# Attention on one Trainium2 core: in even chunks the sum of turns, its rounding and its phases move forward, and GpSimd's tally is cut in two

## What is computed

```python
mag = np.sqrt(a_re * a_re + a_im * a_im)
scale = np.minimum(mag, 0.999) / (mag + 1e-06)
a_re_n, a_im_n = (a_re * scale, a_im * scale)
for t in range(S):                                   # B, H, S, D = 4, 8, 768, 48
    new_re = ar * S_re - ai * S_im                   # ar, ai: a_re_n, a_im_n at t
    new_im = ar * S_im + ai * S_re
    kv = np.einsum('bhd,bhe->bhde', k[:, :, t], v[:, :, t])
    S_re, S_im = (new_re + kv, new_im)
    y[:, :, t] = np.einsum('bhd,bhde->bhe', q[:, :, t], S_re)
...
e_idx = np.argmax(x @ w_gate, axis=1)                # x: y by token, for the experts
eom = 1.0 / (1.0 + np.exp(-(x @ w_output_gate)))     # scales the chosen expert's output
```

## Time and profile before

| | |
|---|---|
| median of 3 runs | 978.09 us (977.53 to 978.83) |
| the profiled execution: its own time | 978.09 us |
| its span in the trace | 976.3 us |
| attention, in the trace | to about 290 us |
| experts and feed-forward | from there to the end |
| PE busy | 940.3 us, 96% of the span |
| DVE, ACT, POOL busy | 438.7, 441.9, 510.1 us |
| granted TensorE clock | 0.996 of full |

### The profile page before, as it was taken

The page is one execution under the profiler, slowest core; times in us unless marked ns, Lnnn a source line. Parts: engine busy times, 40 slices in busy tenths (PEclk is TensorE's granted clock), DMA queues, the critical chain, the costliest instruction groups (busy, mean ns, idle before and its releaser), DMA issues.

```text
span 976.3 us, 18188 instructions
## 1 busy us (share of the span) xinstructions
PE 940.3 (96%) x5904; PEld 836.7 (86%) x5905; DVE 438.7 (45%) x794; ACT 441.9 (45%) x742; POOL 510.1 (52%) x429
## 2 busy tenths in 40 slices
PE   5999999999879999999999999999999999999997
PEld 4777878887877989989999898999998999999997
DVE  5898898898846333433433432222222122222111
ACT  7999888997711222222222333333333333333322
POOL 4134656656464986767759923343243433423433
PEclk9999999999989999999999999999999999999999
DMA  3642363340153645335355520010010000000000
GB/s 121 205 139 83 113 238 99 101 137 2 64 183 94 205 133 167 113 105 169 113 169 169 130 57 17 9 41 17 9 49 17 29 21 17 33 1 1 33 1 32
DMA packets 74123, 83.89 MB, mean 86 GB/s; under 512 B 57653, under 2 KB 63305, under 8 KB 71497
## 3 DMA queue, kind: packets, MB, share of 16 engines
q1 hardware_dynamic: 67048, 47.20, 17.5%
q0 software_dynamic: 6144, 34.65, 10.2%
q10 hardware_dynamic: 864, 1.19, 0.3%
HBM read 65.59 MB, written 17.38 MB: 85 GB/s over the span
## 4 chain that ended last, share of the span: by engine, by line
PE 77%; ACT 10%; DVE 5%; issue 5%; DMA 1%; POOL 1%; ACTq 1%; SPq 0%; POOLq 0%; DVEq 0%
PE bank L2168 21%; PE bank L2181 20%; PE bank L2156 12%; PE bank L2131 12%; PE bank L2141 3%; PE bank L1098 2%; DVE neglog L850 1%; PE bank L1180 1%; PE bank L1138 1%; PE bank L1166 1%; PE bank L1140 1%; PE bank L1108 1%; PE bank L1121 1%; DVE neglog L857 1%; ACT log_sq L643 1%
## 5 line engine op out<-in xcount | busy, mean ns | idle before, releaser
L1922 POOL TENSOR_TENSOR act_r<-act_f,act_r 128x512 fp32r<-128x512 f32 x96 | 124.7, 1298 | 258.2 <-ACT act_r L1984 258.1
L2181 PE MATMUL bank<-w_out_r,act_r 128*128 128x384 f32 x1152 | 216.6, 336 | 0.3 <-POOL act_r L1922 0.3
L2168 PE MATMUL bank<-x,w_in_r 128*128 128x512 f32 x864 | 215.7, 394 | 0.0
L2181 PEld LDWEIGHTS bank<-w_out_r,act_r 128*128 128x128 f32 x1152 | 203.8, 188 | 9.1 <-POOL act_r L1922 0.6
L2063 DVE TENSOR_TENSOR act_f<-bank,small 128x512 f32<-128x512 f32 x96 | 66.5, 692 | 286.9 <-ACT small L1981 286.9
L2168 PEld LDWEIGHTS bank<-x,w_in_r 128*128 128x128 f32 x864 | 160.6, 187 | 30.1
L1981 ACT ACTIVATE small<-bank 128x512 f32<-128x512 f32 x96 | 57.5, 599 | 194.7 <-PE bank L2168 194.5
L2131 PE MATMUL bank<-wm,x_tr 128*128 (+1 forms) x522 | 129.1, 401 | 1.5 <-issue 1.0
L2156 PE MATMUL bank<-wm,h_tr 128*128 (+1 forms) x696 | 125.6, 336 | 0.0
L2156 PEld LDWEIGHTS bank<-wm,h_tr 128*128 128x128 f32 x696 | 121.5, 188 | 2.5
L2131 PEld LDWEIGHTS bank<-wm,x_tr 128*128 128x128 f32 x522 | 96.0, 188 | 23.3 <-issue 2.2
(11 more groups left out here) (195 smaller groups left out, 1363.9 us busy)
## 6 DMA issues: line engine op xcount, KB each, us to landing
stage<-moe_w POOLq DMA_DIRECT2D x12, 1536.0 KB, 7.3
qkv_in<-in_qkv SPq DMA_DIRECT2D x24, 576.0 KB, 6.0
a_in<-in_a SPq DMA_DIRECT2D x11, 768.0 KB, 5.2
stage<-moe_w SPq DMA_DIRECT2D x4, 1536.0 KB, 7.1
x_q<-x_sorted SPq DMA_DIRECT2D x116, 48.0 KB, 1.9
y_sorted<-y_b SPq DMA_DIRECT2D x29, 192.0 KB, 1.9
xg<-y_sorted SPq DMA_DIRECT2D x96, 48.0 KB, 1.9
stage<-w_out POOLq DMA_DIRECT2D x2, 1536.0 KB, 7.0
```

Of the source, the lines that this page charges most:

```text
L1922: pool.tensor_tensor(a[:, 1, :], act_f[f % 2][:, :], a[:, 0, :].bitcast(F32), ALU.subtract).then_inc(s_gl, 1)
L2168: last = pe.matmul(h_bank[f % 2][:, :], w_in_r[:, wp, t * F2 + f * P:t * F2 + (f + 1) * P], window_part(w, xp)[:, t, :], start=(t == 0 and ...
L2181: last = pe.matmul(o_bank[j][:, 0:W], a[:, ap, j * P:(j + 1) * P], w_out_r[:, wp, f * W:(f + 1) * W], start=(f == 0 and n == 0), stop=(f = ...
```

## The change

In even chunks except chunk 0, `sum_turns` stands on PE right behind `scores(n, 1)`, ahead of the two `sum_logs` and of `outputs(n, 0)`; on ACT `rounded` stands behind the table load and ahead of `falls` and of everything else that follows in that chunk, `leading(0)` of chunk 20 included; on DVE `phases` stands ahead of `half_tangent`. On POOL the four instructions that select the output gate's logit leave `tally` and become `output_gate`. In chunks 6, 10, 14 and 18 this is called between `cosine_log` and `sine_eps`, one chunk later than before; in chunks 20, 22 and 24 directly behind `tally`, where they stood. No instruction is added or taken away.

```diff
         def tally(g):
...
             pool.sem_inc(s_acc, 1)
+
+        def output_gate(g):
+
+            high = of_group(lg_all, g, E, 2 * E)
+            best, top, part = by_token(half_sum, g, E // 2), by_token(fourth_sum, g, E // 4), by_token(parts, g, E)
             step(pool.tensor_tensor(part, of_group(pick, g), high, ALU.mult))
             step(pool.tensor_tensor(best, part[:, :, 0:4], part[:, :, 4:8], ALU.add))
             step(pool.tensor_tensor(top, best[:, :, 0:2], best[:, :, 2:4], ALU.add))
...
             u = chain_exp(n)
             if u is not None:
                 cosine_log(u)
+            if n % B == 2 and B < n < NCH - 4:
+                output_gate(n // B - 1)
+            if u is not None:
                 sine_eps(u)
...
                 rows(n - 1)
                 if u is not None:
                     act.preload_act_table_set("exp_and_others")
+                if n > 0:
+                    for m in summed(n):
+                        rounded(m)
                 for m in fallen(n):
                     falls(m)
...
                 if n == NCH:
                     gate_exps(GLAST)
-                for m in summed(n):
-                    rounded(m)
+                if n == 0:
+                    for m in summed(n):
+                        rounded(m)
...
                 u = chain_exp(n)
+                if n > 0:
+                    for m in summed(n):
+                        phases(m)
                 if u is not None:
                     half_tangent(u)
-                for m in summed(n):
-                    phases(m)
...
             scores(n, 1)
             if n == 0:
                 keep_warm(6, s_lnu, 4)
+            if n % 2 == 0 and n > 0:
+                for m in summed(n):
+                    sum_turns(m)
             for m in fallen(n):
                 if m > 3:
                     sum_logs(m)
             outputs(n, 0)
-            if n % 2 == 0:
+            if n == 0:
                 for m in summed(n):
                     sum_turns(m)
```

More of the change, by code:

```diff
@@ L525, in tally @@
             n, size = GROUPS[g]
-            low, high = of_group(lg_all, g, 0, E), of_group(lg_all, g, E, 2 * E)
-            best, top, part = by_token(half_sum, g, E // 2), by_token(fourth_sum, g, E // 4), by_token(parts, g, E)
+            low = of_group(lg_all, g, 0, E)
             if n >= RINGX:
@@ L615, in scan_gpsimd @@
                     tally(g)
+                    output_gate(g)
             if n % B == 2 and 0 <= g < GLAST - 2:
@@ L622, in scan_gpsimd @@
                 tally(GLAST - 1)
+                output_gate(GLAST - 1)
             if n == NCH - 1:
@@ L627, in scan_gpsimd @@
                 tally(GLAST)
+                output_gate(GLAST)
                 gate(GLAST)
```

## The result

The changed kernel takes **973.0 us** (median of 4 runs, 972.04 to 975.16) where the kernel before, run beside it, takes 978.46 (4 runs, 977.53 to 979.72). The ratio is 0.9949, with a 95% interval of 0.9935 to 0.9964: faster by 5.5 us, or by half a per cent.

The account below looks back on a forecast made before the run. The prediction took the attention's loop to be bound by PE. From 978.09 us it took 3.3 for nine filled holes and added 1.2 lost in chunk 20, giving 976.0 us, with a range from 974.7 to 977.6.

Parts of the forecast that it names:

- A hole of h us gives back the smaller of h and 0.71: PE, before the sums of logarithms, even chunks 2 to 18: moved sum of turns fills nine holes, gaining 3.3 us.
- The tally: POOL's split, chunks 6, 10, 14, 18: cosine_log starts up to 0.7 us earlier; alone 1.4 us, beside PE's move nothing.
- DVE's and ACT's moves at nothing: Even chunks to 18: early rounded on ACT and phases on DVE fit into idle or covered time, costing nothing.
- Chunk 20: ACT's rounding ahead of the weight copy waits for the sum of turns: 1.2 us idle, a loss of 1.2 us.
- Rival (1): The holes' gain comes but chunk 20's loss does not: 974.8 us; chance 0.13.
- Rival (2): PE's hole moves to transposes(n + 1, 0) or the sum: 977.6 at half the gain, 979.3 at none; 0.19 with rival (4).
- Rival (3): POOL's four instructions take the port before DVE's cap, delaying decay_log in four chunks: 2.9 us, 978.9; chance 0.06.
- Rival (4): PE's holes are not for want of the logarithms: nothing gained, chunk 20 costs 1.2, 979.3; chance 0.19 with rival (2).
- spread of 0.4 us: Whole-time forecast: 0.4 us allowed around it for the terms' rounding, with a chance of 0.62.

Follow-up runs that it names:

- e2: Kernel before with only GpSimd's tally cut in two parts; median 976.13 us (9 runs), ratio 0.9969.
- e5: Kernel before with six useless transposes of zeros (0.66 us) on PE ahead of the sums of logarithms in even chunks 2 to 18; 979.47 us (1 run).
- e1: Changed kernel with GpSimd's tally in one piece again, where it stood before; median 974.64 us (10 runs), ratio 0.9953 to the kernel before.
- e3: Kernel before with only the sum of turns moved on PE; median 973.32 us (10 runs), ratio 0.9949.
- e6: Changed kernel without its moves on ACT and DVE (PE's move and split tally only); median 972.60 us (4 runs), ratio 0.9935 to the kernel before.
- e4: Kernel before with three useless transposes of zeros (0.33 us) on PE ahead of the sums of logarithms in even chunks 2 to 18; 979.29 us, ratio 0.9994.
- e8: The changed kernel itself run once more; median 974.20 us (4 runs), ratio 0.9953 to the kernel before.

## Why the prediction fell short

**The step that failed: "A hole of h us gives back the smaller of h and 0.71".** The mechanism was right (the holes were filled), and the size of this term was not. The nine holes gave 5.78 us instead of 3.3. The prediction let the two sums of logarithms take 1.56 and the sum of turns 0.71 wherever they stand; in the new order they take 1.29 and 0.65. Filling a hole gave back three things:

- the idle time itself, 0.34 in chunk 10,
- 0.27, by which the products behind the hole take longer (1.56 against 1.29), since their semaphore is not there early enough,
- 0.06, since the sum of turns costs 0.65 behind the scores and 0.71 behind the outputs.

Together 0.67, as measured in chunks 10 and 14. Chunks 12 and 16 with their hole of 0.18 should then give 0.51, and did. In chunk 8 the hole of 0.70 is longer than the sum of turns, and the semaphore still comes only when PE is there. In the changed kernel, DVE's and then PE's timeline:

```profile
119.43 0.97 DVE neglog L871
...
120.45 1.56 PE L1116 MATMUL bank<-neglog,tri 128*128 128x384 f32 x4
```

There the slow start stays and only 0.71 is gained (0.65 of the hole is filled, and 0.06 is the difference of the sum's two places). In chunks 2 and 4 the semaphore's lead is now 0.23 and 0.22, so by the rule they give 0.42 + 0.23 + 0.06 = 0.71 each; chunk 4 did, and chunk 2 gave 0.66. Over all nine the rule makes 0.71 x 3 + 0.67 x 4 + 0.51 x 2 = 5.8, and 5.78 was measured. e2 and e5 gained most of the same extra without this move.

It could have been read beforehand. The prediction took 1.56 for two sums of logarithms and 0.71 for one sum of turns from the earlier trace rows, and these are the same matrix product: two should cost twice what one costs. Instead, 1.56 is 0.26 more than two of 0.65. And in the kernel before, such a product without a wait in front stands in the chain with 0.65:

```profile
243.61 0.65 PE bank L1108 x2
```

**The tally: right in what it does, wrong in its worth.** `cap` was indeed held up by L486 and is freed by the split. In the changed kernel, chunk 10, DVE's timeline and then POOL's:

```profile
138.84 0.70 DVE L864 TENSOR_SCALAR neglog<-log_sq 128x768 f32<-128x768 f32 x1
139.58 0.96 DVE L871 SCALAR_TENSOR_TENSOR neglog<-neglog,eps_mag 128x768 f32<-128x768 f32 x1
...
137.30 1.82 POOL L486 TENSOR_TENSOR main<-main,log_sq 128x768 f32<-128x768 f32 x1 [1.46 <-ACT main L654]
139.09 0.57 POOL L544 TENSOR_TENSOR parts<-pick,lg_all 128x32 f32<-128x32 f32 x1
139.74 0.88 POOL L545 TENSOR_TENSOR half_sum<-parts 128x16 f32<-128x16 f32 x1
```

L486 starts as soon as ACT's logarithm is there, at 137.30, which is 3.53 us ahead of the end of the scores instead of 2.95 (144.39 - 141.44): 0.58 earlier, where "up to 0.7" was forecast. `cap` ends at 139.54, 0.42 behind L486's end at 139.12, and that is the same 0.42 as in the earlier trace rows. It still waits for L486, only for less: 0.28 us of overlap instead of 0.86. In chunk 12 of the kernel before L486 ended at 164.15 and `cap` at 164.57, 0.42 again. The lag is 0.41 to 0.43 for each of the ten `cap` from 35 us on in before, the changed kernel, e1 and e2, while the rows' own lengths run from 0.66 to 2.12 us. So, by estimate, `cap` itself takes 0.42 and the rest of its row is the wait. That agrees with the rule of the Trainium skill that the prediction cited ("SBUF — State Buffer", "Who interferes with whom"). It isn't the split as such that makes `cap` short, but the earlier end of L486. Alone this gives 2.35 us, not 1.4, again by the leads. Beside the other move I had it give nothing; it gives 0.5 (200.71 against 201.23), since it keeps `qr` early enough for the transposes (e1).

**DVE's and ACT's moves at nothing: right** in the even chunks to 18, by e3 against e1 (0.02 us) and e6 against the change (0.02). In the changed kernel's timeline of ACT the rounding fits in where ACT was idle, `falls` follows it, and the copy of queries still waits for PE:

```profile
141.51 0.58 ACT L682 ACTIVATE whole<-bank,rounder 128x384 f32<-128x384 f32 x1 [0.21 <-PE bank L1126]
142.16 0.49 ACT L676 ACTIVATE fall<-bank 128x384 f32<-128x384 f32 x1
145.51 0.59 ACT L708 ACTIVATE q_t<-bank 96x512 f32<-96x512 f32 x1 [0.77 <-PE bank L1158]
```

**Chunk 20: right.** Forecast was an idle time of 1.2 us of ACT and a loss of 1.2; it was 1.07 idle, and 1.0 to 1.1 lost between the second and the third mark (18.74 against 17.72 and 17.65). No other wait took it up. All runs with ACT's early rounding have the loss (18.74, 18.76 and, with one more, 19.91), and none without it has (17.44 to 17.72).

**The rivals.** Rival (1), no loss in chunk 20, is refuted by these rows. Rival (2), the hole that moves, did not come in chunks 2 to 18: the waits for `qr` before the transposes are what they were (5.1 us in 11 times, and 5.2 in 11 before), and PE's one new wait for ACT is the 1.29 us of chunk 20, which was forecast as ACT's loss. Behind chunk 22 a wait of 1.3 us before the scores is new as well, while one of 1.5 for `x_t` shrinks to 0.3; from the third mark to the next copy `x_t` it is 16.4 us in both kernels, so that costs nothing. Rival (3), POOL's four instructions ahead of `cap`, did not come either: `cap` ends 0.42 behind L486 with L544 queued behind it as without, and L545, which took 0.22 in e1, takes 0.88 beside `decay_log`: it was POOL that was held up, not DVE. Rival (4) is refuted by the nine holes.

**The sum with the measured terms** is 978.09 - 5.8 + 1.1 = 973.4, and 973.0 and 974.2 were measured. The prediction's spread of 0.4 us had taken the rounding of the terms alone into account; the price of a hole was read in the one view that shows idle time, and no bound was set on it.

**Where the profiled execution's own 2.9 us come from.** At the start of the experts it was ahead by 5.5: about 0.8 from the first transfers, ahead of chunk 0 and no doing of the change, 5.8 from the stretch, less 1.0 for chunk 20. It lost 1.3 again between 298.5 and 305.7, where the granted clock was 0.76, and 1.2 in one wait of the experts. In the windows (stretch, length, busy us of PE, PEld, DVE, ACT and POOL, granted clock, DMA share and GB/s), PE's timeline and the waits:

```profile
298.50:305.70 7.20, 6.36 (x23) 4.95 (x24) 2.98 (x8) 1.09 (x2) 5.73 (x2) 0.76 0.17 32
...
299.87 5.96 PE L2152 MATMUL bank<-wm,x_tr 128*128 x18 [0.84 <-issue]
...
PE bank L2177 <- DVE h_tr L2061: 1.2, 1, 1.2
```

The same 18 products took 4.46 us in the kernel before. The other three executions beside it took 972.04 to 973.44; they have no trace, but are faster by about as much.

## What to carry to other kernels

Price a wait of PE by comparing the products behind it with the same products where none waits, not by the idle time that the profile prints: here 0.34 us of idle time cost 0.67, and a semaphore that was in time by 0.06 us still cost 0.14. Useful work whose operands are old belongs in front of a product that waits, but on an in-order engine that has slack only by luck (ACT in chunk 20) the same move can uncover a wait that a long copy used to hide; move it on the engine that is the bound and leave the others alone.

## What the runs showed of the hardware

A matrix product whose semaphore comes just when PE does costs 0.27 us more than one whose semaphore is 0.3 us ahead, though PE is not idle in either (e4: 1.56 with 0.01 us of idle time; e5: 1.29). Before a transpose the same cost 0.14 (e1).

A VectorE instruction on 128x768 numbers (`cap`) ended 0.42 us behind the end of the GpSimd instruction (L486) that was under way when it started, whether its own row was 0.66 or 2.12 us long. The profile shows no idle time there, so the wait is in the row.

The granted clock fell to half in differing places of the thin stretch from 250 to 310 us, where PE waits more often. Every profile has such a fall (1.2 instead of 2.4 GHz) at the end of the attention, between 274 and 293 us, the shortest in e3 and the longest in e4. In e8 it was 0.60 from 256 to 260 us, so for most of it at 1.2 instead of 2.4 GHz, after PE had stood idle for 1.29 and 1.54 us in chunks 21 and 22. Windows, then PE's and ACT's timelines of e8:

```profile
256.00:260.00 4.00, 4.00 (x29) 3.20 (x28) 3.48 (x3) 3.01 (x4) 3.40 (x2) 0.60 0.00 0
...
248.41 1.13 PE L1139 MATMUL bank<-q_t,k_t 96*128 96x128 f32 x8 [1.29 <-ACT q_t L708]
...
255.61 0.33 PE L1156 MATMUL bank<-ident,qr 128*96 128x128 f32 x1 [1.54 <-DVE qr L927]
...
259.36 0.60 ACT L722 ACTIVATE x_t<-bank 128x512 f32<-128x512 f32 x1 [0.81 <-PE bank L1189]
```

It lost 1.2 us there: 19.91 from the second mark to the third, with 18.74 in the other execution of the same kernel. That one had the same waits, 1.29 and 1.55 us, and a clock of 1.00 from 256 to 260, so the waits alone do not bring the fall. In the profile of e4 the clock was 0.50 all the way from 278 to 290 us (0.72 in before, after and e8), and in that of after it fell a second time at 298.5. Runs of one kernel spread by 1.5 us and more to either side of their median, so a change of 1 us is told far better by the profile's stretches than by the whole time of a few runs. Whether the 1.29 us of chunk 20 make such a fall more likely is open: two profiles of the changed kernel are too few, and in e1, which has that loss too, the clock stayed at 1.00 there.
